# The scores of a head pair as two products of 64 rows and 72 columns, from the third chunk on

## The reference

```python
k_p = k.reshape(B, H, S // 8, 8, D).mean(axis=3)       # pooled keys, 72 for each head
v_p = v.reshape(B, H, S // 8, 8, D).mean(axis=3)
scores = q @ k_p.transpose(0, 1, 3, 2) / sqrt(D)
attn = exp(scores - max(scores)); attn /= (sum(attn) + 1e-9)
x = heads_side_by_side(attn @ v_p)                       # 4608 tokens x 512
h = x @ moe_w_in                                         # 512 -> 2048, an activation, then moe_w_out
x = act1(h) @ moe_w_out
out = relu(x @ moe2_w_in) ** 2 @ moe2_w_out
```

## Time and profile before

| | |
|---|---|
| median of 3 runs | 1576.48 us (1576.22 to 1576.88) |
| the profiled execution | 1576.08 us |
| its span, first to last instruction | 1574.3 us |
| PE busy / weight loads busy | 99% / 98% |
| DVE / ACT / POOL busy | 73% / 55% / 16% |
| first scores pass of unit 8, last of unit 47 | at 64.5 us, at 471.7 us |

### The profile page before, as it was taken

One profiled execution on the slowest core, in us unless ns is written; L12 is line 12 of the kernel. 1 busy time (PEld: TensorE's weight loads), 2 busy tenths in 40 slices (PEclk: granted clock), 3 DMA queues, 4 the chain that ended last, 5 costly groups with the idle time before them and its releaser, 6 DMA issues.

```text
span 1574.3 us, 25577 instructions
## 1 busy us (share of the span) xinstructions
PE 1565.2 (99%) x9173; PEld 1548.1 (98%) x9173; DVE 1146.3 (73%) x1883; ACT 861.7 (55%) x1608; POOL 247.8 (16%) x356
## 2 busy tenths in 40 slices
PE   8999999999999999999999999999999999999999
PEld 6999999999999999999999999999999999999999
DVE  7777667677666867877879777666667986876874
ACT  5777678767676644444445654444456643443442
POOL 7645338725500000000000000000000000000000
PEclk9999999999999999999999999999999999999999
DMA  8366469557537544344244642442448645245231
GB/s 286 105 225 229 172 208 327 188 198 231 187 123 231 170 161 142 100 161 146 96 161 153 235 146 96 161 151 103 148 157 290 194 150 192 80 140 186 91 116 41
DMA packets 173951, 262.80 MB, mean 167 GB/s; under 512 B 16640, under 2 KB 153856, under 8 KB 173824
## 3 DMA queue, kind: packets, MB, share of 16 engines
q1 hardware_dynamic: 173824, 261.16, 49.7%
HBM read 154.14 MB, written 106.95 MB: 166 GB/s over the span
## 4 chain that ended last, share of the span: by engine, by line
PE 95%; DVE 2%; ACT 1%; issue 1%; DMA 0%; POOL 0%; DVEq 0%; POOLq 0%; ACTq 0%
PE bank L854 42%; PE bank L726 25%; PE bank L877 22%; PE bank L686 2%; PE bank L697 1%; DVE gf L1290 1%; DVE b L1283 1%; PE bank L716 1%; PE bank L718 1%; PE bank L717 1%; PE bank L715 1%; DVE f_lo L1258 0%; PE bank L701 0%; DMA k_raw<-k 0%; ACT pT_rest L931 0%
## 5 line engine op out<-in xcount | busy, mean ns | idle before, releaser
L854 PE MATMUL bank<-gf,f_hi 128*128 128x384 f32 x2688 | 682.6, 334 | 0.5 <-DVE u_b L1300 0.4
L854 PEld LDWEIGHTS bank<-gf,f_hi 128*128 128x128 f32 x2688 | 485.3, 188 | 1.3 <-DVE u_b L1300 0.9
L854 PE MATMUL bank<-gf,f_lo 128*128 128x384 f32 x1344 | 448.9, 334 | 0.0
L990 ACT ACTIVATE gf<-b 128x768 fp32r<-128x768 f32 x336 | 278.5, 845 | 263.1 <-PE bank L854 174.1
L1290 DVE TENSOR_TENSOR gf<-b,gf 128x768 fp32r<-128x768 f32 x336 | 314.4, 951 | 43.4 <-ACT gf L990 43.4
L877 PE MATMUL bank<-xf,w_hi 128*128 128x384 f32 x1344 | 340.8, 334 | 0.0
L726 PE MATMUL bank<-x_hi,wi_hi 128*128 128x384 f32 x752 | 260.1, 346 | 0.5 <-DVE g_st L1371 0.5
L854 PEld LDWEIGHTS bank<-gf,f_lo 128*128 128x128 f32 x1344 | 252.3, 188 | 0.0
L726 PE MATMUL bank<-x_hi,wi_lo 128*128 128x384 f32 x752 | 252.2, 335 | 0.0
L726 PE MATMUL bank<-x_lo,wi_hi 128*128 128x384 f32 x752 | 252.2, 335 | 0.0
L877 PEld LDWEIGHTS bank<-xf,w_hi 128*128 128x128 f32 x1344 | 242.4, 188 | 0.0
(11 more groups left out here) (103 smaller groups left out, 1499.7 us busy)
## 6 DMA issues: line engine op xcount, KB each, us to landing
b<-g_dram SPq DMA_DIRECT2D x192, 384.0 KB, 4.1
g_dram<-g_st SPq DMA_DIRECT2D x192, 192.0 KB, 2.3
g_dram<-c_st SPq DMA_DIRECT2D x192, 192.0 KB, 1.9
s_dram<-su_s SPq DMA_DIRECT2D x24, 512.0 KB, 2.9
k_raw<-k SPq DMA_DIRECT2D x32, 288.0 KB, 3.5
q_sb<-q SPq DMA_DIRECT2D x48, 192.0 KB, 2.8
y_dram<-o_st SPq DMA_DIRECT2D x48, 192.0 KB, 1.9
x_raw<-y_dram SPq DMA_DIRECT2D x24, 384.0 KB, 5.4
```

Of the source, the lines that this page charges most:

```text
L854: last = mm(dst[:, 0:H], w[:, 2 * i + kt, cols], x[:, half, kt, :], start=q_ < 3 and i == 0 and kt == 0 and h == 0, stop=q_ >= 4 and i == ...
L990: copy(gf[layer][r % GRING][:, 0], unit_source(n)[:, 2 * i:2 * i + 2, :], ACT.Copy).then_inc(gf_hi, 1)
```

## The change

From unit 8 on (`HEADS_APART = 2 * HP`), the product of 128 rows and 144 columns becomes two products of 64 rows and 72 columns, one for each head. The first head's go to bank 3 and the second head's to bank 4, which are now one tensor, `twin`. Since both banks are written at once, the scores wait for `s_prob` to reach a, where they waited for `s_below` to reach a - 1. DVE's maximum and subtraction read both banks through one access pattern with one dimension more. The zeros in `kT` stay, but from unit 8 on they aren't read.

```diff
+    HEADS_APART = 2 * HP
...
+        twin = ctx.enter_context(nc.psum_tensor("twin", [P, 2, 512], F32))
+        bank += [twin[:, n] for n in range(2)]
...
             def scores(a):
                 pe.wait_ge(q_in[a % QRING], 16 * (a // QRING + 1))
                 pe.wait_ge(k_ready, keys_of(a))
-                if a >= 2:
+                if a >= HEADS_APART:
+                    pe.wait_ge(s_prob, a)
+                elif a >= 2:
                     pe.wait_ge(s_below, a - 1)
...
-                        if m0 < m1:
-                            last = mm(s_ps[a % 2][m0 - t * P:m1 - t * P, t * KEYS:(t + 1) * KEYS],
+                        if m0 >= m1:
+                            continue
+                        tokens = slice(m0 - t * P, m1 - t * P)
+                        if a < HEADS_APART:
+                            last = mm(s_ps[a % 2][tokens, t * KEYS:(t + 1) * KEYS],
                                       q_sb[a % QRING][:, m0:m1], kT[:, m % KRING, :], start=True, stop=True)
+                            continue
+                        for h in range(2):
+                            rows = slice(h * Dh, (h + 1) * Dh)
+                            last = mm(s_ps[h][tokens, t * G:(t + 1) * G], q_sb[a % QRING][rows, m0:m1],
+                                      kT[rows, m % KRING, h * G:(h + 1) * G], start=True, stop=True)
                 last.then_inc(s_full, 1)
...
+            def score_views(a):
+
+                if a < HEADS_APART:
+                    return (s_ps[a % 2][:, 0:NT * KEYS].rearrange("p (n k) -> p n k", k=G),
+                            by_head(prob[a % 2][:, :, :]), top[:, :])
+                return (twin[:, :, 0:NT * G].rearrange("p h (t k) -> p t h k", k=G),
+                        prob[a % 2][:, :, :].rearrange("p t (h k) -> p t h k", h=2),
+                        top[:, :].rearrange("p (t h) -> p t h", h=2))
...
             def below(a):
 
-                src = s_ps[a % 2][:, 0:NT * KEYS].rearrange("p (n k) -> p n k", k=G)
+                src, dst, most = score_views(a)
                 dve.wait_ge(s_full, a + 1)
                 if a:
                     dve.wait_ge(s_below, a)
-                vec.tensor_reduce(top[:, :], src, AX_X, ALU.max).then_inc(s_top, 1)
+                vec.tensor_reduce(most, src, AX_X, ALU.max).then_inc(s_top, 1)
                 dve.wait_ge(s_top, a + 1)
                 if a >= 2:
                     dve.wait_ge(t_full, a - 1)
-                vec.tensor_tensor(by_head(prob[a % 2][:, :, :]), src,
-                                  top[:, :].unsqueeze(2).broadcast_to([P, 2 * NT, G]), ALU.subtract)\
-                    .then_inc(s_below, 1)
+                most = most.unsqueeze(len(src.shape) - 1)
+                vec.tensor_tensor(dst, src, most.broadcast_to(src.shape), ALU.subtract).then_inc(s_below, 1)
```

## The result

The changed kernel takes 1586.46 us (1586.21 to 1586.94, 4 runs) against 1576.35 us (1576.14 to 1576.88, 4 runs) for the kernel before on the same chip: +10.1 us, a ratio of 1.0064 with a 95% interval of 1.0047 to 1.0081. It is slower by 0.64%.

A forecast was written before the change was run, and what follows sets the result against it. The prediction took PE to bound the kernel between 64 and 472 us. Adding 7.4 + 1.6 = +9.0 us to the profiled 1576.08 gave 1585.1, and 0.4 for the median gave 1585.5 us; own range 1582 to 1591, 80% range 1574 to 1604.

The forecast's parts named there:

- The bound: Between 64 and 472 us, time that PE loses or gains is lost or gained at the kernel's end.
- the 1.0 and 1.2: Sign on the chain: scores with about 1.0 us per three-block unit and 1.2 us per four-piece unit.
- Half rows side by side, loads as the pace: Scores on PE: both heads' half-row products run at once, each step bound by its load, 0.1085 us.
- rival 4: Scores on PE: the two heads' loads follow one another, about +36 us, 1612.5 us; chance 12%.
- The crossing: Each change of array shape around the scores costs about 0.093 us of nothing, then an uncovered load, 0.054 or 0.107.
- rivals 1 and 2: Scores' crossing: 1, free for half rows, 1567.5 us, chance 8%; 2, array drains, loads not held up, 1575 us, chance 12%.
- Loads under passes within a half: Scores on half rows: loads hide under the pass before, so steps follow at 0.1085 us.
- rival 3: Scores: within half of the rows a load waits for the pass before, 0.17 us a step, 1596 us; chance 10%.
- The new wait at zero: The scores' wait for s_prob costs nothing, since the transposes ahead on PE wait for the same count.
- DVE at zero: DVE's two instructions with the extra pattern dimension keep their duration, about 0.6 us each, and cost zero.
- The sum: Scores on PE: +7.4 us for 28 three-block units and +1.6 us for 12 four-piece units, +9.0 us in all.

The follow-up runs named there:

- the first experiment: The kernel before with only the new wait added, the scores from unit 8 on waiting for s_prob to reach a: 1576.1 us, ratio 0.9997.
- quarters: The changed kernel with every scores product cut in two again by tokens (64 rows, 64 stationary, 72 moving columns, four side by side): 1572.99 us, ratio 0.9979.
- the three versions: Against the kernel before: middle block of four-piece units as one product, 1572.57 us; quarters everywhere, 1572.99 us; quarters only in four-piece units, 1572.29 us.
- quarters where a batch ends: Quarters in the 12 units of four pieces alone, the 28 units of three blocks with the products of the kernel before: 1572.29 us, ratio 0.9975.

## Why the prediction was right

- **The bound**, that PE's time between 64 and 472 us is the kernel's time: right. A unit's distance grew by 10.55 - 10.24 = 0.31 us for three blocks and by 10.97 - 10.80 = 0.17 for four pieces. 28 x 0.31 + 12 x 0.17 = 10.7 us, from two distances rounded to 0.01, against +10.3 in the span. On the chain the scores stand with 0.82 and 1.04 us and not with the 1.0 and 1.2 that I had named as a sign, since the 0.2 of the way back is counted behind them.
- **Half rows side by side, loads as the pace**: right. It rested on a row about half columns and was the open point of the prediction. The pairs of loads show it, and the version with both heads on the same rows cost 24.4 us more where I had 25. This takes rival 4 away.
- **The crossing**: right in kind and in size. From the last full pass's end at 309.92 to the load at 310.02 it is 0.10 us with the half rows, and from 310.97 to 311.06 on the way back 0.09, where I had taken 0.093 from half columns. The load behind it is not hidden: the first L742 pass and the load ahead of it take 0.28 us together (332.59 to 332.87 below), where a pass alone takes 0.17. This takes rivals 1 and 2 away.
- **Loads under passes within a half**: the pairs are 0.11 us apart and not 0.17, so rival 3 falls. The Trainium skill ("TensorE: Matmul & The Clock Gate", Part 3) has the rule that a load overlaps a pass only where the row groups differ. The trace disagrees for half rows as for full ones: pairs of the same two halves follow each other 0.11 us apart, at the pace of the loads. The promise of up to 2x in the Trainium skill ("TensorEngine Tiling (Array Packing)", Overview) didn't come true either: the kernel lost 10.1 us. The Trainium skill says on the same page, under Key Properties, that changing the mode drains TensorE. The idle 0.25 us on PEld agrees.
- **The new wait at zero** and **DVE at zero**: both right, by the first experiment and by the 608 and 601 ns.
- **The sum**, +9.0 against a measured +10.1: each unit was a little small. I had 0.265 for three blocks and it is about 0.31, and 0.13 for four pieces where it is about 0.17. The starts of full products around unit 33 show where the rest sits. The changed kernel has these:

```profile
331.50 0.34 PE L742 MATMUL bank<-x_hi,wi_lo 128*128 128x384 f32 x1
...
332.59 0.44 PE L742 MATMUL bank<-x_hi,wi_hi 128*128 128x384 f32 x1
332.87 0.34 PE L742 MATMUL bank<-x_lo,wi_hi 128*128 128x384 f32 x1
...
334.81 0.33 PE L731 MATMUL bank<-pT_hi,v_hi 128*128 128x384 f32 x1
```

And the kernel before had these:

```profile
325.24 0.33 PE L726 MATMUL bank<-x_hi,wi_lo 128*128 128x384 f32 x1
...
326.33 0.34 PE L726 MATMUL bank<-x_lo,wi_hi 128*128 128x384 f32 x1
...
328.24 0.33 PE L715 MATMUL bank<-pT_hi,v_hi 128*128 128x384 f32 x1
```

From the last full product ahead of the scores to the second one behind them it is 332.87 - 331.50 = 1.37 us against 326.33 - 325.24 = 1.09, so +0.28 in place of my 0.265. The slot's products behind that take 1.94 us against 1.91, another 0.03, which the prediction left out. The means over all 28 such units in the two traces are +0.29 and +0.02. With both heads on the same rows the products behind take 1.91 us as before. Why they take longer in the changed kernel stays open.

## What to carry to other kernels

Where PE is the bound, cost a smaller product by the longer of its weight load and its pass, and then add the way in and the way out of the new shape: here 0.1 us of nothing each, plus a load that no pass hides, some 0.35 us in all. A shape that wins 0.014 us a step, six times, can't pay for that. Once the crossing is paid anyhow, as in the units where a batch ends, go on to the shape that fills the array best: quarters made such a unit 0.33 us shorter, where halves of the rows made it 0.17 longer. And look at the chain again after each gain: 3 to 4 us below the kernel before, it already left PE in two of the three versions.

## What the runs showed of the hardware

The way in costs the same for every shape tried: the weight loads idle 0.25 us before the first load of half columns, half rows and quarters alike. I had reckoned with that, but no row of before showed it for half rows or quarters. 24 loads and 24 passes of quarters fit in about 0.5 us, so on this stream the number of instructions was no limit. What the prediction hadn't counted are the full products behind the way back, which take 0.02 to 0.03 us a slot more than before. And the shapes tried for the scores span 39 us of the kernel's time, from 1572.3 (quarters where a batch ends) to 1610.9 (half rows, both products on the same half, which leaves out the second head's scores).
